# Attention by pairs of tokens and in half-row tiles, with the last groups placed between the first expert products

## What is computed

```python
for c in range(nc):                       # 24 chunks of 32 tokens
    q_c = q[:, :, c_start:c_end]
    k_full = np.concatenate([mem_k, k_ctx], axis=2)     # 8 + at most 56 keys
    v_full = np.concatenate([mem_v, v_ctx], axis=2)
    scores = scale * np.matmul(q_c, k_full.transpose(0, 1, 3, 2))
    scores = scores - np.max(scores, axis=-1, keepdims=True)
    a = np.exp(scores)
    a = a / (np.sum(a, axis=-1, keepdims=True) + 1e-09)
    out[:, :, c_start:c_end] = np.matmul(a, v_full)
# x: [1536, 512]; mixture 1 has 4 experts, mixture 2 has 8 (gates by a Sinkhorn iteration)
for e in range(E):
    h = np.maximum(x @ w1[e], 0.0)        # 512 -> 1024
    out += p[:, e:e + 1] * (h @ w2[e])    # 1024 -> 512
```

## Time and profile before

| what | value |
|---|---|
| median of 3 runs | 1660.2 us (1655.78 to 1661.17) |
| time of the profiled execution | 1659.28 us |
| its span, first to last instruction | 1657.4 us |
| mean granted TensorE clock | 0.979 of full |
| busy: TensorE, VectorE, ScalarE, GpSimd | 96%, 54%, 41%, 39% |
| first product of quad 0, first down product | 104.0 us, 141.1 us |

### The profile page before, as it was taken

The page is one execution under the profiler, slowest core; times in us unless marked ns, Lnnn a source line. Parts: engine busy times, 40 slices in busy tenths (PEclk is TensorE's granted clock), DMA queues, the critical chain, the costliest instruction groups (busy, mean ns, idle before and its releaser), DMA issues.

```text
span 1657.4 us, 21410 instructions
## 1 busy us (share of the span) xinstructions
PE 1589.5 (96%) x8692; PEld 1441.1 (87%) x8692; DVE 903.0 (54%) x1342; ACT 684.7 (41%) x1058; POOL 647.1 (39%) x517
## 2 busy tenths in 40 slices
PE   7648999989999999999999999998999999999999
PEld 6648998979998988989989989988999999999997
DVE  5535555564555564675555555556555555555553
ACT  5534434443434444344344344344433443443441
POOL 2314343443243453333433433444334334334331
PEclk9879999999999999999999999999999999999999
DMA  9832222221122121112221221221222122122121
GB/s 173 128 70 66 75 64 65 76 64 51 52 89 61 54 89 52 51 51 64 89 61 54 89 63 52 89 64 51 89 89 64 53 88 64 55 86 64 56 85 39
DMA packets 158931, 117.76 MB, mean 71 GB/s; under 512 B 31336, under 2 KB 129640, under 8 KB 158832
## 3 DMA queue, kind: packets, MB, share of 16 engines
q1 hardware_dynamic: 158832, 116.39, 25.3%
HBM read 113.22 MB, written 3.15 MB: 70 GB/s over the span
## 4 chain that ended last, share of the span: by engine, by line
PE 88%; DVE 4%; SPq 4%; ACT 2%; issue 1%; DMA 1%; ACTq 0%; DVEq 0%
PE banks L446 29%; PE banks L448 29%; PE banks L447 29%; DVE t_lo L779 2%; SPq L236 1%; SPq L235 1%; DVE s_lo L774 1%; PE banks L520 1%; DVE banks L787 1%; DMA v_bd<-in_mem_v 1%; ACT s_hi L638 1%; ACT h_hi L660 0%; ACT part L656 0%; SPq L238 0%; DVE rows L809 0%
## 5 line engine op out<-in xcount | busy, mean ns | idle before, releaser
L368 POOL TENSOR_TENSOR w_lo<-w_raw,w_hi 128x1024 fp32r<-128x1024 f32 x96 | 317.3, 3305 | 751.9 <-ACT w_hi L643 751.9
L446 PE MATMUL banks<-t_lo,s_hi 128*128 128x384 f32 x1344 | 459.2, 342 | 24.5 <-ACT part L656 13.5
L448 PE MATMUL banks<-t_hi,s_lo 128*128 128x384 f32 x1344 | 456.3, 340 | 0.0
L447 PE MATMUL banks<-t_hi,s_hi 128*128 128x384 f32 x1344 | 455.8, 339 | 0.0
L446 PE MATMUL banks<-w_lo,h_hi 128*128 128x512 f32 x1152 | 449.8, 390 | 0.0
L447 PE MATMUL banks<-w_hi,h_hi 128*128 128x512 f32 x1152 | 449.3, 390 | 0.0
L448 PE MATMUL banks<-w_hi,h_lo 128*128 128x512 f32 x1152 | 448.9, 390 | 0.0
L656 ACT ACTIVATE part<-banks 128x384 f32<-128x384 f32 x384 | 188.4, 493 | 624.9 <-PE banks L448 624.7
L787 DVE TENSOR_TENSOR banks<-banks,part 128x384 f32<-128x384 f32 x384 | 207.1, 561 | 326.0 <-ACT part L656 190.8
L660 ACT ACTIVATE h_hi<-banks 128x384 fp32r<-128x384 f32 x384 | 186.6, 492 | 261.9 <-DVE banks L787 261.9
L446 PEld LDWEIGHTS banks<-t_lo,s_hi 128*128 128x128 f32 x1344 | 256.9, 191 | 31.7 <-issue 13.3
(11 more groups left out here) (92 smaller groups left out, 640.7 us busy)
## 6 DMA issues: line engine op xcount, KB each, us to landing
w_raw<-in_moe_w SPq DMA_DIRECT2D x192, 256.0 KB, 3.2
w_raw<-in_moe_w SPq DMA_DIRECT2D x48, 1024.0 KB, 5.5
v_bd<-in_v SPq DMA_DIRECT2D x16, 308.0 KB
w_raw<-in_q SPq DMA_DIRECT2D x8, 384.0 KB, 5.1
k_in<-in_k SPq DMA_DIRECT2D x8, 384.0 KB
out_x<-rows SPq DMA_DIRECT2D x12, 256.0 KB, 2.7
v_bd<-in_mem_v SPq DMA_DIRECT2D x16, 48.0 KB
v_bd<-in_v SPq DMA_DIRECT2D x16, 10.0 KB
```

Of the source, the lines that this page charges most:

```text
L368: pool.tensor_tensor(out=w2_lo[m % 2][:, fs, :], in0=w2_raw[:, fs, :], in1=w2_hi[m % 2][:, fs, :].bitcast(F32), op=ALU.subtract).then_inc( ...
L446: pe.matmul(out_, lhs_hi, rhs_lo, start=start, stop=False, skip_group_check=chained)
L447: pe.matmul(out_, lhs_hi, rhs_hi, start=False, stop=False, skip_group_check=chained)
L448: return pe.matmul(out_, lhs_lo, rhs_hi, start=False, stop=stop, skip_group_check=chained)
```

## The change

Two units become a group `g` of four heads, worked off in halves `hf` of 384 tokens. Keys and values are held as pairs of tokens: `v_t` holds a pair (512 bytes) to a partition, 32 pairs for each head and chunk, and `k_t` is the turned keys without the block-diagonal copy, so ScalarE does all of `copy_k` in one instruction. `scores` addresses a 64x32 tile of the array for each head and chunk (48 products of 56 columns) and takes the 8 memory keys in 12 products of 8 columns on 64x128 tiles. `attend` takes 48 products of 128 columns on 64x32 tiles for half a row of a group, and the row sums in 6 products of 4 columns with `head_of` on the whole array. `q_in` and `k_in` have one buffer instead of two, GpSimd puts the keys in order too, and `turn_q(u)` and its neighbours share other banks. The last 16 `keep_busy` transposes are gone. Groups 2 and 3 (the second batch) stand between the products of quads 0 and 1, and product (0, 0) waits for the first batch alone. At the changes of pass, `next_tokens` stand earlier in the orders of ScalarE and VectorE, and ScalarE's `split_w2` comes behind them. The low part of the first `w2` goes from GpSimd to VectorE. `shift` and `scale_x` keep their steps: two small memsets, a reduction, now two subtractions of 128x384 instead of one of 128x768; an addition, a reciprocal and two products. The diff, cut:

```diff
+        GROUPS = UNITS // 2
+        q_ps = [banks[0] if u < 6 else banks[2] for u in range(UNITS)]
+        k_ps = [banks[1] if u < 6 else banks[2] for u in range(UNITS)]
+        s_ps = [banks[2] if u < 6 else banks[3] for u in range(UNITS)]
+        pt_ps = [banks[0] if g < 2 else banks[2] for g in range(GROUPS)]
+        xt_ps = [banks[1] if g < 2 else banks[2] for g in range(GROUPS)]
+        po_ps = banks[3]
...
+            def load_v(g, hf):
+                if g:
+                    sp.wait_ge(att_out, 2 * (g - 1) + hf + 1)
                 else:
-                    sp.wait_ge(v_bd_zeroed, u + 1)
...
+                    sp.wait_ge(v_zeroed[hf], 1)
+                chunks = slice(hf * HC, (hf + 1) * HC)
+                for h in range(4):
+                    vh, mv = v[g // 2, 4 * (g % 2) + h], mem_v[g // 2, 4 * (g % 2) + h]
+                    at, dst = h * KEYS // 2, v_t[:, :, h % 2, :, :].rearrange("p c a d -> p c (a d)")
+                    first = at + MEMP
+                    c0 = 1 if hf == 0 else HC
+                    windows = bass.AP(tensor=vh.tensor, offset=vh.offset + (c0 * CHUNK - LEFT) * D,
+                                      ap=[[2 * D, FULL], [CHUNK * D, HC - 1], [1, 2 * D]])
+                    sp.dma_start(dst[first:first + FULL, c0:c0 + HC - 1, :], windows).then_inc(v_loaded[hf], 16)
...
+                    memory = bass.AP(tensor=mv.tensor, offset=mv.offset, ap=[[2 * D, MEMP], [0, HC], [1, 2 * D]])
+                    sp.dma_start(dst[at:at + MEMP, chunks, :], memory).then_inc(v_loaded[hf], 16)
...
+            for g in range(GROUPS):
+                load_v(g, 0)
+                if g < GROUPS - 1:
+                    load_qk(2 * g + 2)
+                load_v(g, 1)
+                if g < GROUPS - 1:
+                    load_qk(2 * g + 3)
+                if g == 0:
                     load_w1(0)
-                if u == 4:
...
+                if g == 1:
...
+            def order(u):
+                pool.wait_ge(q_loaded, 16 * (u + 1))
                 pool.wait_ge(q_turned, u)
-                pool.tensor_copy(q_rows[:].rearrange("p r h d -> p h r d"), q_in[u % 2]).then_inc(q_ordered, 1)
+                pool.tensor_copy(q_rows[:].rearrange("p r h d -> p h r d"), q_in).then_inc(q_ordered, 1)
+                pool.wait_ge(k_loaded, 32 * (u + 1))
+                pool.wait_ge(k_turned, u)
+                pool.tensor_copy(k_rows[:].rearrange("p r h d -> p h r d"), k_in).then_inc(k_ordered, 1)
...
+            for u in range(1, 4):
+                order(u)
+            sum_s(0)
+            order(4)
+            sum_t1(0)
+            order(5)
+            order(6)
+            sum_t23(0)
+            sum_t4(0)
+            order(7)
+            sum_s(1)
...
                 for c in range(NC):
                     t, j = c // 4, c % 4
-                    mm = pe.matmul(s_ps[j * CHUNK:(j + 1) * CHUNK, t * P:(t + 1) * P],
-                                   q_t[u % 2][:, c * CHUNK:(c + 1) * CHUNK], k_bd[:, c, :], start=True, stop=True,
-                                   tile_position=(0, j * CHUNK))
+                    for h in range(2):
+                        hs = slice(h * D, (h + 1) * D)
+                        to = s_ps[u][j * CHUNK:(j + 1) * CHUNK, h * 512 + t * KEYS:h * 512 + (t + 1) * KEYS]
+                        pe.matmul(to.rearrange("p (a k) -> p a k", a=2)[:, :, MEMP:MEMP + FULL],
+                                  q_t[u % 2][hs, c * CHUNK:(c + 1) * CHUNK],
+                                  k_t[hs, :, c * CHUNK // 2:c * CHUNK // 2 + FULL], start=True, stop=True,
+                                  tile_position=(h * D, j * CHUNK))
+                for t in range(ST):
+                    for h in range(2):
+                        hs = slice(h * D, (h + 1) * D)
+                        to = s_ps[u][:, h * 512 + t * KEYS:h * 512 + (t + 1) * KEYS]
+                        mm = pe.matmul(to.rearrange("p (a k) -> p a k", a=2)[:, :, 0:MEMP],
+                                       q_t[u % 2][hs, t * P:(t + 1) * P], k_t[hs, :, KPAIRS - MEMP:KPAIRS],
+                                       start=True, stop=True, tile_position=(h * D, 0))
                 mm.then_inc(scores_ready, 1)
...
+            def attend(g, hf):
+                n = 2 * g + hf
+                pe.wait_ge(pt_ready, n + 1)
...
+                pe.wait_ge(v_loaded[hf], 16 * V_DMAS * (g + 1))
+                for t in range(3):
+                    for a in range(2):
+                        for j in range(4):
+                            for r in range(2):
+                                hs = slice(r * D, (r + 1) * D)
+                                pe.matmul(po_ps[j * CHUNK:(j + 1) * CHUNK, r * 512 + t * P:r * 512 + (t + 1) * P],
+                                          p_t[hs, a, t * P + j * CHUNK:t * P + (j + 1) * CHUNK],
+                                          v_t[hs, hf * HC + 4 * t + j, :, a, :], start=a == 0, stop=a == 1,
+                                          tile_position=(r * D, j * CHUNK))
+                for t in range(3):
+                    for a in range(2):
+                        mm = pe.matmul(po_ps[:, 3 * P + 4 * t:3 * P + 4 * t + 4], p_t[:, a, t * P:(t + 1) * P],
+                                       head_of[:], start=a == 0, stop=a == 1)
                 mm.then_inc(att_out, 1)
...
             scores(0)
             turn_q(1)
             turn_k(1)
-            pe.wait_ge(shifted, 1)
-            keep_busy(WARMUPS[2])
             scores(1)
...
+            for g in range(2):
+                turn_q(2 * g + 2)
+                turn_k(2 * g + 2)
+                turn_probs(g, 0)
+                scores(2 * g + 2)
+                attend(g, 0)
+                turn_q(2 * g + 3)
+                turn_k(2 * g + 3)
+                turn_probs(g, 1)
+                turn_x(g, 0)
+                scores(2 * g + 3)
+                attend(g, 1)
+                turn_x(g, 1)
+            turn_q(6)
+            turn_k(6)
+            product(0, 0)
+            turn_probs(2, 0)
+            product(0, 1)
+            scores(6)
+            attend(2, 0)
+            product(0, 2)
+            turn_q(7)
+            turn_k(7)
+            product(0, 3)
+            turn_x(2, 0)
+            product(0, 4)
+            turn_probs(2, 1)
+            scores(7)
+            product(0, 5)
+            attend(2, 1)
+            product(0, 6)
+            turn_x(2, 1)
+            product(1, 0)
+            turn_probs(3, 0)
+            product(1, 1)
+            attend(3, 0)
+            product(1, 2)
+            product(1, 3)
+            turn_x(3, 0)
+            product(1, 4)
+            turn_probs(3, 1)
+            attend(3, 1)
+            product(1, 5)
+            product(1, 6)
+            turn_x(3, 1)
+            for quad in range(2, ALLQ):
...
                 keep_part(quad, 0)
                 next_tokens(quad, 0)
                 take_turned(quad, 1)
-                next_tokens(quad, 1)
                 take_turned(quad, 2)
                 hidden(quad, 0)
                 keep_part(quad, 1)
+                next_tokens(quad, 1)
                 take_turned(quad, 3)
                 keep_part(quad, 2)
+                next_tokens(quad, 2)
                 take_turned(quad, 4)
                 keep_part(quad, 3)
+                next_tokens(quad, 3)
                 take_turned(quad, 5)
                 hidden(quad, 1)
                 take_turned(quad, 6)
...
                 hidden(quad, 3)
                 if quad + 1 < ALLQ:
                     split_s(quad + 1)
+                for i in range(4, PRODUCTS):
+                    next_tokens(quad, i)
                 split_w2(quad // 2, quad % 2)
-                for i in range(2, PRODUCTS):
-                    next_tokens(quad, i)
...
             shift(0)
-            copy_k(1)
             shift(1)
...
+            for g in range(2):
+                shift(2 * g + 2)
+                scale_x(g, 0)
+                if g == 1:
                     gate_of_first_mixture()
                     split_s(0)
...
+                    split_t(0, 0)
+                    split_t(0, 3)
+                shift(2 * g + 3)
+                scale_x(g, 1)
+            split_t(0, 1)
+            split_t(0, 2)
+            add(0, 0)
+            shift(6)
+            hidden(0, 0)
+            scale_x(2, 0)
+            split_t(0, 4)
+            split_t(0, 5)
+            split_t(0, 6)
+            split_s(1)
+            add(0, 1)
+            shift(7)
+            add(0, 2)
+            hidden(0, 1)
+            scale_x(2, 1)
+            add(0, 3)
+            hidden(0, 2)
+            hidden(0, 3)
+            add(1, 0)
+            hidden(1, 0)
+            scale_x(3, 0)
+            add(1, 1)
+            hidden(1, 1)
+            scale_x(3, 1)
+            add(1, 2)
+            hidden(1, 2)
+            add(1, 3)
+            hidden(1, 3)
+            split_s(2)
+            split_w2(0, 0)
+            split_w2(0, 1)
```

(109 more changed lines are left out.)

415 lines of the change are left out of this document (195 added, 220 removed).

## The result

The changed kernel takes 1680.0 us (median of 4, 1677.7 to 1680.5) beside 1658.0 (median of 4) for the kernel before on the same chip: 1.0135 times as long, 95% interval 1.011 to 1.0159. Slower, as forecast, but by 22 us where 7 were forecast.

The account below looks back on a forecast made before the run. It took the values' DMA to bound the attention, then TensorE's own chain after the change; 1659.3 + 18.5 (later D) - 12 (changes of pass) = 1665.8, as a median 1667 us; range 1643 to 1690.

Parts of the forecast that it names:

- D: Moment of the first down product, behind the attention and quads 0 and 1; forecast 159.6 us, 18.5 later than 141.07.
- the clock's term: Half clock up to D: 5 us, as 1.5 and 1.8 around two stalls and 1.7 for the small products.
- TensorE's queue at full clock: TensorE's work from its start until product (2, 0), without stalls: 117.6 us.
- S + A: Time of one `scores` (S, 4.8 us) plus one `attend` (A, 3.7 us) in the attention.
- stalls for which something is awaited: TensorE's waits for other engines and loads until product (2, 0): 29.6 us in all.
- rival 1: Small tiles in the attention are cheap: S = 3.7, A = 3.2, D = 146.6, total about 1654 us; chance 0.34.
- rival 2: Clock at half for much of the attention: some 25 us in place of 3.5, total 1688; chance 0.15.
- The wait of `turn_q(6)`: In the attention, unit 6's queries come late behind `load_w1(1)` and 12 value DMAs: 4.1 us, until 81.3.
- Values' DMAs: In the attention, `attend`'s waits for value loads, 28.4 us before, nearly gone; DMA stops being the bound.
- The changes of pass: Moving two splits at the changes of pass wins 4.0 us, three times: 12 us, bounds 6 and 19.
- rival 3: Changes of pass win little, `w_lo` hitting a later split: 4 us instead of 12, total 1675; chance 0.11.
- three signs set down beforehand: Forecast wrong if S + A is below 7, the first 150 us' clock below 0.8, or D before 150.

Follow-up runs that it names:

- e4: The changed kernel with 289 spare transposes added where TensorE would idle and beside the small products; 1.0072 of the kernel before.
- e1: The kernel before with only next_tokens and split_w2 ordered on ScalarE and VectorE as in the change; 0.9966 of the kernel before, 5.6 us less.
- e11: The changed kernel with load_w1(1) one group later and most memory products and row sums left out; 1659.0 us in one execution.

## Why the prediction was off

The direction was right, and TensorE's own chain does take the place of the DMAs; but that it came out longer than before is in part luck. At full clock the chain is 24 us shorter than forecast, and with the stalls as measured D would stand near 133 (93.6 + 32.0 + 7.35), ahead of the 141.1 before. Half clock and standstills made it longer: two errors of opposite sign, 24 us and 26.5, all but cancel. The size was not right: 22 us where 7 were forecast. The **step that failed is the clock's term**, "I count 5 us". It allowed half clock around two stalls, for 1.8 and 1.5 us, and 1.7 for the small products. What the runs showed in its place: the clock fell seven times, behind waits and standstills alike, and stood at half for 90 of the first 160 us; TensorE was at work in 69 of them, and that cost some 30 us. Product (2, 0) was forecast for 147.2 at full clock and started at 160.44. By the steps:

| term | predicted | measured |
|---|---|---|
| TensorE's queue at full clock | 117.6, with S + A = 8.5 | 93.6: S + A = 5.5 takes 8 x 3.0 off |
| stalls for which something is awaited | 29.6 | 32.0 |
| standstills without a wait | 0 | 4.8 |
| half clock ahead of product (2, 0) | 3.5 of the 5 | 30.0, what is left of 160.44 |
| from there to D | 7.35 + 1.5 | 9.85 |
| D | 159.6 | 170.3 |

The stalls are the idle time up to 160.44, 38.3 us (TensorE was busy for 122.17), less 1.5 at the start and the 4.8. The clock's 30 us are a remainder and hold the errors of the other terms. Two things bear them out: the starts of every group of instructions against those of the same group at full clock add up to some 33 us, and e4, with the clock at 0.94 to 1.00, has D at 151.3 with 289 transposes more.

- *S and A*: too dear by 3.0 us, and past the point (7.1) where rival 1 was to decide. The rival's saving was real, 24 us and more than its 13, and the 27 ns of the earlier trace rows were not the instruction's: the 96 take 1.06 us in `scores` and 1.52 in `attend`, nearer the 0.6 and 1.3 of streaming alone than the 2.6. The Trainium skill ("TensorE: Matmul & The Clock Gate", "Wait — 56ns, not 53.3ns?") has a floor of about 25 ns from start to start; the rows at 42.94 and 45.44 go below it, at 11 and 16. Of the small products, those of `scores` cost 60 ns instead of 92, the row sums 113. The 92 was too low for 128-column loads: it divides 1 us by a window's count of 11, which takes in instructions that run across its edges. But the time did not end where rival 1 had it, since half clock and the standstills took more than the 24 us back.
- *The clock*: rival 2, held at 0.15, came true in effect, with its 25 us in place of 3.5 near the 30 measured, though not for the reason given: it argued from a run of few-column products, and the falls stand in or behind idle time. The argument against it misread the trace of before. There it was not one `attend` that ran at half clock but five of the eight, each behind 3.1 us of waiting or more:

```profile
30.43 2.39 PEld L432 LDWEIGHTS banks<-v_bd,p_t 128*32 128x32 f32 x48 [3.32 <-issue]
...
40.40 2.39 PEld L432 LDWEIGHTS banks<-v_bd,p_t 128*32 128x32 f32 x48 [3.27 <-issue]
...
61.12 2.40 PEld L432 LDWEIGHTS banks<-v_bd,p_t 128*32 128x32 f32 x48 [3.36 <-issue]
...
97.72 2.40 PEld L432 LDWEIGHTS banks<-v_bd,p_t 128*32 128x32 f32 x48 [13.43 <-issue]
```

  With the fifth, in the earlier trace rows, they are all the `attend` with such a wait; the three at full clock waited 2.1 us or less. So the stalls of the attention were followed by work at half clock in the kernel before too, yet the forecast had 23.4 us of stalls ahead of product (2, 0)'s own and priced the clock at one of them. Two rivals came true at once, of opposite sign; the forecast gave each its own time and never their sum.
- *The wait of* `turn_q(6)`: right in place and cause; 5.9 us for 4.1, at 88.7 instead of 81.3. `turn_q(2)`, 4.5 us, was not foreseen: twelve DMAs ahead of its queries fill the engines.
- *The other waits*: `turn_x(0, 1)` 1.6 for 1.7, `turn_x(1, 1)` 5.4 for 2.8, `attend(2, 0)` and `attend(2, 1)` 2.5 and 1.5 for 2.5 and 1.8, product (2, 0) for its split 5.7 for 6.2.
- *Values' DMAs*: right, no wait is left.
- *The changes of pass*, the other term of the sum that was mis-sized: 7.9 us won behind D, 5.6 by e1, for 12. The waits for `part` are 10.2 us for the predicted 6. Splits still take 2.63 us at 370 us, beside a subtraction of GpSimd, and 3.91 for two at 381, beside `w_lo`. This is rival 3's mechanism in part.
- Of the three signs set down beforehand, two showed: S + A below 7 (5.5) and a clock below 0.8 in the first 150 us (0.70). They pull in opposite directions.

What stays open: whether the small products keep the clock at half longer once it has fallen. No fall lies in them, and e11 without most of them has no higher clock, but it also idles more.

## What to carry to other kernels

Splitting a product into tiles makes TensorE's arithmetic cheap and its instruction stream dear: look at how many instructions a microsecond the stream must bring, and at what the granted clock does behind every stall of the trace at hand, before nanoseconds at full clock are added up. A busy share near 100% at a clock of 0.50 is a stall that no list of waits shows. And when a stall is a queue held by one waiting load, move the load first: here that and an order of splits gave 1.1%, where the rewriting, which holds the same order, lost 1.35%.

## What the runs showed of the hardware

- Tile products on 64x32 tiles issue every 10 to 12 ns at 56 columns and every 16 at 128, at full clock; at half clock every 15 and 31.
- A long run of them (1,152) stops after every 128 matmuls for 1.5 to 3.3 us once the first 247 are through, one of 384 after its first 149: the instruction queue's packets of 16 KB come 3.3 to 4 us apart.
- 8-column products on 64x128 tiles take 56 ns at full clock and 107 at half; within a run of 240 the clock fell, and it came back only in the products of 384 columns behind it. 120 transposes of 128 columns hold the full clock.
- In the changed kernel's attention the clock fell seven times ahead of product (2, 0), six times within idle stretches of 1.6 to 5.7 us or at their end, the seventh 1.9 us behind a standstill of 1.4.
